# Two slot tiles ahead of the last batch's routing, in an attention, expert and mixing kernel

## The chip, the cores and the metric

The kernel runs on one core of a Trainium2 chip. The metric is the device time of one execution in microseconds (us), as the median of several runs. The engines are named as in the profile: PE (TensorE) multiplies matrices, DVE (VectorE), ACT (ScalarE) and POOL (GpSimd) work on elements, SP (SyncE) only issues transfers. All of them run side by side and wait for one another by semaphores. "PEq", "SPq" and the like are their instruction queues.

## The reference: what is computed

Three stages follow one another on 4 batches of 576 tokens.

```
attention (8 heads of 64):  scores = q k^T / 8;  keep scores >= row maximum - tau;  softmax;  times v
x = heads side by side                                       # 2304 tokens x 512
experts:  logits = x @ w_gate;  e = argmax, or the token before's e while the local gate is >= 0.5 (in one batch)
          out = softmax(logits)[e] * (relu(x @ w1[e]) @ w2[e])          # 8 experts, 512 -> 1024 -> 512
mixing:   theta = x @ w_theta;  zr, zi = x cos, x sin;  y = w_tok_r zr + w_tok_i zi;  u = x + y
          out = u + relu(u @ w_ch)
```

A token goes to exactly one expert. With the reference's inputs the eight experts get 521, 178, 345, 351, 172, 172, 227 and 338 tokens; 354 of expert 0's 521 are in the first three batches. In tiles of 128 rows that is 5, 2, 3, 3, 2, 2, 2 and 3 tiles, 22 in all.

## The kernel before

**Attention** works on 16 pairs of heads (0 to 15, four a batch), each in nine tiles of 128 query rows. In a pair, PE makes the scores, DVE takes row maxima (L417) and masks (L432), ACT the exponentials (L686), DVE the reciprocals of the row sums for three tiles at a time (`recip`, L447), POOL scales those tiles (`norm`, L339), PE turns them (L581) and multiplies by v (L604). Each engine has its order written out by hand in its `pair` function. In the last pairs POOL also splits expert 0's weights, 1024 columns at a time, into a high and a low part (`split_piece`, L65 and L67; the calls are the `pieces` of the last `pair` calls).

**Routing** (`route`) turns the gate's logits into places. Tokens are sorted by expert; each expert gets whole tiles ("slot tiles") of 128 rows. The first three batches are routed during pair 15 (`fresh`, `rows`, `follow`, `count`, `places` with argument 0, then `early`), the last batch after attention (the same with argument 1, then `tile_numbers`, `next_tile`, `next_source`, `all_tiles`, `sources`, `tables`, `weights`). DVE does nearly all of it in one chain; PE has short hops (`rows_pe`, `experts_pe`, `ranks_pe`, and `slots_pe`, 15 or 20 small matmuls that give the token number for each lane of one or more tiles). `hot_lane`, a 128x128 tile for each of 20 groups of tokens, is made by DVE for the first `OWN_LANES` groups and by POOL for the others (`lanes`).

Tile 0 is filled from the first three batches alone, so it can be worked on while the last batch is still being routed. Its rows are fetched from `x_dram` by an indirect DMA of POOL (`fetch`, L1278) with the numbers in `ahead`. Tile 1 is fetched with the second column of `ahead`, after `next_source`; tile 2 with `source`, which `sources` writes for all tiles. The other 23 slots (3 to 25, empty ones too) are gathered by POOL into `stage`, ten places in turn (`gather`), and written by SP to `xs_dram` (L1235), one after another: SP waits for each write to land before it issues the next (L1234). PE's tiles read them back through ACT (L1423).

**Experts** (`experts`): a tile is `transposes_x`, `up` (24 matmuls, L1365), `transposes_h` (L1374), `down` (24 matmuls, L1387). Weights of expert e lie in one of two halves of `w_split`. Expert 0's are split during attention, expert 1's by ACT and DVE (`high`, `low`) beside the first tiles. Experts 2 to 7 are split by POOL in `split` (L1267 high part, L1270 low part): four pieces for `up`, four for `down`, 8 pieces an expert. POOL reaches them only when its 23 gathers are issued. SP loads the raw pieces: expert 2's first four (L1210) before the writes to `xs_dram`, expert 2's last four (L1213) and all others after those writes. From tile 1 on a loop runs: `transposes_h(j)`, `up(j+1)`, `transposes_x(j+2)`, `down(j)`.

**Mixing** is a block of its own; all engines meet ahead of it.

## Time and profile before

| what | us |
|---|---|
| median of 3 runs | 868.75 (868.54 to 869.04) |
| the profiled execution, its own time | 867.34 |
| its span, first to last instruction | 865.6 |
| PE busy | 814.1 (94% of the span) |
| POOL busy | 509.6 (59%) |
| DVE busy | 461.3 (53%) |
| ACT busy | 389.3 (45%) |

In the span attention takes 0 to about 309, the experts 309 to 609, mixing 609 to the end. PE is the busiest engine throughout, so the questions are where it waits, and at which of its two clocks it runs. A busy time says nothing of which wait ends last: for that one reads the bracket at a row's end ("[idle before <-releaser]").

### The profile page before, as it was taken

What the parts mean: (1) busy time and instruction counts of PE and PEld (TensorE: products, weight loads), DVE (VectorE), ACT (ScalarE), POOL (GpSimd) and SP (SyncE); (2) the same over time, 40 slices, a digit from 0 to 9 for tenths busy, and PEclk for the clock granted to TensorE, in tenths of its full rate; (3) what the DMA queues carried; (4) which work ended last, traced back from release to release, by engine and by line L of the source; (5) the groups of instructions that cost most, each with busy time, mean ns of one, the idle gap of its engine ahead of it and who ended that gap; (6) DMA issues with size and microseconds to landing.
All of it is one profiled execution on the core that took longest, in us unless ns stands there. A gap on an engine that the chain in (4) does not pass through costs nothing. (4 is left out here: it accounts for less than half of the span.)

```text
span 865.6 us, 16405 instructions
## 1 busy us (share of the span) xinstructions
PE 814.1 (94%) x5087; PEld 682.8 (79%) x5088; DVE 461.3 (53%) x1078; ACT 389.3 (45%) x669; POOL 509.6 (59%) x464
## 2 busy tenths in 40 slices
PE   6969999999999889999999999998489999999998
PEld 3758878888887657888888888886367899998998
DVE  5748888888888867222122212211286746636622
ACT  2748878787887543221122112121375525434310
POOL 4536776676689837254989999995285605313100
PEclk7879999999999988999999999999699999999999
DMA  6976777768756167765655655650310111100101
GB/s 178 349 177 173 179 190 192 192 170 192 202 129 182 60 220 253 232 208 196 204 196 168 194 179 174 207 193 24 115 49 19 44 56 28 55 28 1 49 9 55
DMA packets 78982, 123.77 MB, mean 143 GB/s; under 512 B 26336, under 2 KB 39904, under 8 KB 78944
## 3 DMA queue, kind: packets, MB, share of 16 engines
q1 hardware_dynamic: 69200, 100.47, 39.9%
q0 software_dynamic: 3552, 11.54, 4.5%
q10 hardware_dynamic: 6192, 11.27, 4.0%
q8 instruction: 21, 0.34, 0.2%
q14 instruction: 17, 0.14, 0.0%
HBM read 70.63 MB, written 24.12 MB: 109 GB/s over the span
## 5 line engine op out<-in xcount | busy, mean ns | idle before, releaser
L339 POOL TENSOR_SCALAR p_ring<-p_ring,xs_nat 128x576 f32<-128x576 f32 x144 | 106.1, 752 | 81.2 <-DVE xs_nat L447 81.2
L417 DVE TENSOR_REDUCE xs_nat<-psum 128x1 f32<-128x576 f32 x144 | 106.0, 750 | 45.6 <-PE psum L546 38.1
L546 PE MATMUL psum<-k_st,q_st 128*128 128x288 f32 x600 | 116.6, 321 | 7.2 <-issue 7.1
L432 DVE SCALAR_TENSOR_TENSOR p_ring<-psum,xs_nat,e_ring 128x576 f32<-128x576 f32 x144 | 114.6, 812 | 16.0 <-PE psum L592 11.4
L1387 PE MATMUL psum<-w_split,h_hi 128*128 (+1 forms) x352 | 118.8, 409 | 3.4 <-DVE h_lo L1484 3.2
L1365 PE MATMUL psum<-w_split,x_hi 128*128 (+1 forms) x352 | 117.0, 403 | 1.3 <-DVE x_lo L1479 0.8
L1270 POOL TENSOR_TENSOR w_split<-w_raw,w_split 128x1024 fp32r<-128x1024 f32 x48 | 115.1, 2397 | 4.0
L686 ACT ACTIVATE e_ring<-psum,xs_nat 128x576 f32<-128x576 f32 x144 | 105.6, 750 | 16.0 <-DVE xs_nat L417 15.1
L704 ACT COPY p_t<-psum 128x512 f32<-128x512 f32 x144 | 84.4, 587 | 37.7 <-PE psum L581 34.6
L546 PEld LDWEIGHTS psum<-k_st,q_st 128*128 128x128 f32 x600 | 86.8, 195 | 18.0 <-DVE p_ring L432 10.4
L1638 POOL TENSOR_TENSOR stage<-g,xs_nat 128x512 f32<-128x512 f32 (+1 forms) x20 | 27.4, 1368 | 110.0 <-ACT xs_nat L1844 110.0
L581 PE MATMUL psum<-ident,p_ring 128*128 128x128 f32 x576 | 89.5, 280 | 1.3 <-POOL p_ring L339 0.6
L1771 PE MATMUL psum<-tok_hi,z_hi 128*128 128x288 f32 x288 | 86.3, 300 | 1.4 <-DVE z_lo L1681 1.4
L1771 PE MATMUL psum<-tok_hi,z_lo 128*128 128x288 f32 x288 | 85.1, 296 | 0.0
L1771 PE MATMUL psum<-tok_lo,z_hi 128*128 128x288 f32 x288 | 85.1, 295 | 0.0
L1387 PEld LDWEIGHTS psum<-w_split,h_hi 128*128 128x128 f32 x352 | 67.9, 193 | 19.4 <-issue 3.7
L1365 PEld LDWEIGHTS psum<-w_split,x_hi 128*128 128x128 f32 x352 | 66.6, 189 | 17.0 <-issue 1.8
L1435 ACT CAST h_hi<-psum 128x1024 fp32r<-128x1024 f32 x22 | 22.4, 1016 | 127.7 <-PE psum L1374 125.3
L581 PEld LDWEIGHTS psum<-ident,p_ring 128*128 128x128 f32 x576 | 69.7, 143 | 9.9 <-issue 7.2
L1387 PE MATMUL psum<-w_split,h_lo 128*128 (+1 forms) x176 | 71.1, 404 | 0.0
L1365 PE MATMUL psum<-w_split,x_lo 128*128 (+1 forms) x176 | 70.0, 398 | 0.0
L604 PE MATMUL psum<-p_t,v_sb 128*64 128x256 f32 (+1 forms) x512 | 69.4, 412 | 0.0
(195 smaller groups left out, 1585.6 us busy)
## 6 DMA issues: line engine op xcount, KB each, us to landing
w_raw<-w_dram SPq DMA_DIRECT2D x48, 512.0 KB
k_st<-k_split SPq DMA_DIRECT2D x60, 320.0 KB, 5.4
q_st<-q_split SPq DMA_DIRECT2D x60, 144.0 KB, 2.5
xs_dram<-stage SPq DMA_DIRECT2D x23, 256.0 KB
ys_dram<-y_nat ACTq DMA_DIRECT2D x22, 256.0 KB
xs_nat<-xs_dram ACTq DMA_DIRECT2D x21, 256.0 KB, 3.3
k_nat<-k_t_dram SPq DMA_DIRECT2D x15, 320.0 KB, 4.2
out_dram<-out_sb SPq DMA_DIRECT2D x32, 144.0 KB, 1.8
```

What stands on the lines that cost most here:

```text
L339: pl.tensor_scalar(t, t, rsum[:, col:col + 1], 1.0, ALU.mult, ALU.mult).then_inc(s_norm, 1)
L417: dve.tensor_reduce(negmax[:, u % 3, 0:1], s_bank[u % 3][:, :, 0:HALF], AX.XY, ALU.max, negate=True).then_inc(s_max, 1)
L432: dve.scalar_tensor_tensor(out=p_tile[u].rearrange("p (a b) -> p a b", a=2), in0=s_bank[u % 3][:, :, 0:HALF], scalar=thresh[:, u % 3:u % 3 ...
L546: mm = pe.matmul(bank[:, x, 0:HALF], lhs, key[:, HALF * x:HALF * x + HALF], start=(j == 0), stop=(j == len(terms) - 1))
L581: mm = pe.transpose(bank[:, t * P:t * P + P], keys[:, t * P:t * P + P], ident[:])
L604: mm = pe.matmul(bank[D * h:D * h + D, 0:COLS[a]], v_sb[m % 2][:, h, t, :], moving, start=(t == 0), stop=(t == KT - 1))
L686: act.activation(e_ring[:, u % 3, :].rearrange("p (a b) -> p a b", a=2), s_bank[u % 3][:, :, 0:HALF], ACT.Exp, bias=negmax[:, u % 3, 0:1], ...
L704: act.copy(dst, src).then_inc(s_free, 1)
L1270: lo = pl.tensor_tensor(w_lo[:, (m + 1) % 2, r // 4, part], raw[:, r % 4, :], w_hi[:, (m + 1) % 2, r // 4, part].bitcast(F32), ALU.subtract)
L1365: mm = pe.matmul(ph[:, half, :], a[:, c, :], rhs.rearrange("p o n -> p (o n)"), start=(n == 0), stop=(n == len(terms) - 1))
L1387: mm = pe.matmul(py, a[:, f, :], rhs.rearrange("p o n -> p (o n)"), start=(n == 0), stop=(n == len(terms) - 1))
L1771: mm = pe.matmul(mix_bank(b, q), a[:, k, c * P:c * P + P], w[:, k, half], start=(t == 0 and i == 0), stop=(t == ST - 1 and i == len(terms) ...
```

## The change

`FIRST_TILES` is 2: tiles 0 and 1 are both filled from the first three batches, both of expert 0 (`first` and `put_first` get a last dimension of 2, `ahead` a third column, expert 0 is padded up to 256 early rows where it has fewer). The token numbers of both come from one hop, and POOL issues both fetches one behind the other. Slot tiles grow from 26 to 27, those fetched directly from 3 to 4, so 23 are still gathered. PE now does both halves of `up(1)` between the hops of the last batch; the hop `next` stands behind the first half of `up(1)`, the hop `sources` behind 12 of the 24 matmuls of `down(0)`. DVE, ACT and the loop (from tile 2 now) follow that order; `tables` comes ahead of `sources` on DVE, and ACT makes the high parts of pieces 2 to 4 of expert 1 ahead of `relu(1)`.

In pair 15 DVE's `fresh` and `rows` of the first three batches stand ahead of the masks of tiles 5 and 6 instead of behind `recip(15, 1)`. POOL's `constants` (three short instructions) stand ahead of a weight piece instead of behind the norms. `OWN_LANES` is 10 instead of 8.

```diff
-SLOTS = (BATCH * SEQ + P - EXPERTS) // P + EXPERTS
+FIRST_TILES = 2
+SLOTS = (BATCH * SEQ + FIRST_TILES * P - EXPERTS) // P + EXPERTS
...
+            if p == PAIRS - 2:
+                routing["pool"]["constants"](pl)
             piece(2)
...
             piece(1)
-            if p == PAIRS - 2:
-                routing["pool"]["constants"](pl)
...
                 row_thresh(i, m, 6)
+                if isinstance(i, int) and 2 * i + m == PAIRS - 1:
+                    routing["vector"]["fresh"](dve, 0)
+                    routing["vector"]["rows"](dve, 0)
                 mask(i, m, 5)
                 mask(i, m, 6)
                 sum_eps(i, m, 1)
                 row_thresh(i, m, 7)
                 recip(i, m, 1)
-                if isinstance(i, int) and 2 * i + m == PAIRS - 1:
-                    routing["vector"]["fresh"](dve, 0)
-                    routing["vector"]["rows"](dve, 0)
...
-    OWN_LANES = 8
+    OWN_LANES = 10
...
-        link(v, v.scalar_tensor_tensor(out=first[:], in0=tile_i[:, 0:EARLY_TT], scalar=0.0, in1=hot[0][:, 0, :],
-                                       op0=ALU.is_equal, op1=ALU.mult))
+        for j in range(FIRST_TILES):
+            link(v, v.scalar_tensor_tensor(out=first[:, :, j], in0=tile_i[:, 0:EARLY_TT], scalar=float(j), in1=hot[0][:, 0, :],
+                                           op0=ALU.is_equal, op1=ALU.mult))
...
-    DIRECT = 3
+    DIRECT = FIRST_TILES + 2
...
-        fetch(x_first, keep["ahead"][:, 0:1], EARLY).then_inc(s_first[0], 16)
+        for j in range(FIRST_TILES):
+            fetch(direct[j], keep["ahead"][:, j:j + 1], EARLY).then_inc(s_first[j], 16)
...
         up(0, halves=range(1), part=range(0, 6))
         hop["experts"](pe, 1)
-        up(0, halves=range(1), part=range(6, 10), ready=False)
+        up(0, halves=range(1), part=range(6, 12), ready=False)
         hop["ranks"](pe, 1)
-        up(0, halves=range(1), part=range(10, 12), ready=False)
         up(0, halves=range(1, 2), ready=False).then_inc(s_up, 1)
+        transposes_x(1, direct[1], s_first[1])
+        transposes_h(0)
+        up(1, halves=range(1))
         hop["next"](pe)
-        transposes_h(0)
+        up(1, halves=range(1, 2), ready=False).then_inc(s_up, 1)
+        down(0, part=range(0, 12))
         hop["sources"](pe)
-        down(0, part=range(0, 4))
-        transposes_x(1, xs[:, 1, :], s_first[1])
-        down(0, part=range(4, 24), ready=False).then_inc(s_done, 1)
+        down(0, part=range(12, 24), ready=False).then_inc(s_done, 1)
+        transposes_x(2, direct[2], s_first[2])
+        transposes_h(1)
         reached(pe, "tables")
-        up(1).then_inc(s_up, 1)
-        transposes_x(2, xs[:, 0, :], s_first[2])
+        up(2).then_inc(s_up, 1)
+        transposes_x(3, direct[3], s_first[3])
+        down(1).then_inc(s_done, 1)
         last = rounds(pe)
-        with pe.Fori(1, last) as j:
+        with pe.Fori(2, last) as j:
```

DVE in pair 15, before (L417 row maximum, L422 threshold, L432 mask, L442 and L447 row sums and reciprocals, L912 to L927 the routing steps):

```order
L422 TENSOR_REDUCE xs_nat<-xs_nat 128x1
L432 SCALAR_TENSOR_TENSOR p_ring,xs_nat<-psum,xs_nat,e_ring 128x576 x2
L442 TENSOR_REDUCE xs_nat<-xs_nat 128x3
L422 TENSOR_REDUCE xs_nat<-xs_nat 128x1
L447 RECIPROCAL xs_nat<-xs_nat 128x3
L913 TENSOR_REDUCE top<-logits 128x15
L914 TENSOR_TENSOR stage<-logits,top 128x120
L916 TENSOR_TENSOR stage<-stage,route_const 128x120
L918 TENSOR_REDUCE fe<-stage 128x15
L924 SCALAR_TENSOR_TENSOR held<-logits,route_const 128x3x5
L927 SCALAR_TENSOR_TENSOR held<-held,fe 128x3x5
L417 TENSOR_REDUCE xs_nat<-psum 128x1
```

The same place in the changed kernel (its lines are one higher):

```order
L423 TENSOR_REDUCE xs_nat<-xs_nat 128x1
L914 TENSOR_REDUCE top<-logits 128x15
L915 TENSOR_TENSOR stage<-logits,top 128x120
L917 TENSOR_TENSOR stage<-stage,route_const 128x120
L919 TENSOR_REDUCE fe<-stage 128x15
L925 SCALAR_TENSOR_TENSOR held<-logits,route_const 128x3x5
L928 SCALAR_TENSOR_TENSOR held<-held,fe 128x3x5
L433 SCALAR_TENSOR_TENSOR p_ring,xs_nat<-psum,xs_nat,e_ring 128x576 x2
L443 TENSOR_REDUCE xs_nat<-xs_nat 128x3
L423 TENSOR_REDUCE xs_nat<-xs_nat 128x1
L448 RECIPROCAL xs_nat<-xs_nat 128x3
L418 TENSOR_REDUCE xs_nat<-psum 128x1
```

Six routing instructions moved ahead of two masks and of the reciprocals for which POOL waits.

PE behind `ranks`, before (L1108 the hops' small matmuls, L1344 the x transposes, L1374 the h transposes, L1365 `up`, L1387 `down`):

```order
L1365 MATMUL psum<-w_split,x_hi 128x512
L1108 MATMUL psum<-put_next,hot_lane 128x2 x20
L1374 MATMUL psum<-ident,h 128x128 x8
L1108 MATMUL psum<-put,hot_lane 128x52 x20
L1387 MATMUL psum<-w_split,h_hi 128x512
...
L1344 MATMUL psum<-ident,xs_nat 128x128 x4
```

The same stretch in the changed kernel (between rows left out stand only more matmuls of the kind above them):

```order
L1355 MATMUL psum<-ident,u 128x128 x4
L1385 MATMUL psum<-ident,h 128x128 x8
L1376 MATMUL psum<-w_split,x_hi 128x512
...
L1116 MATMUL psum<-put_next,hot_lane 128x2 x20
L1376 MATMUL psum<-w_split,x_hi 128x512
...
L1398 MATMUL psum<-w_split,h_hi 128x512
...
L1116 MATMUL psum<-put,hot_lane 128x54 x20
L1398 MATMUL psum<-w_split,h_hi 128x512
...
L1355 MATMUL psum<-ident,xs_nat 128x128 x4
L1385 MATMUL psum<-ident,h 128x128 x8
```

The hop of `put_next` moved behind half of `up(1)`, that of `put` behind all of `up(1)` and half of `down(0)`.

DVE behind the last batch's ranks, before (`put` goes into the hop `sources`, `source` is what comes out of it, `need` is the last of `tables`):

```order
L1033 TENSOR_SCALAR put<-here,route_const 128x20x26
L1484 TENSOR_TENSOR h_lo<-psum,h_hi 128x1024
L994 COPY units<-psum 128x26
L995 SCALAR_TENSOR_TENSOR source<-psum,units 128x26
L1039 TENSOR_TENSOR full<-route_const,ends 1x216
L1041 TENSOR_REDUCE units_row<-full 1x27
L1042 TENSOR_SCALAR slot_expert<-units_row 1x27
L1043 TENSOR_SCALAR rounds<-ends 1x1
L1044 MEMSET need 1x9
L1045 TENSOR_SCALAR need<-ends 1x7
L1479 TENSOR_TENSOR x_lo<-psum,x_hi 128x512
```

The same steps in the changed kernel:

```order
L1041 TENSOR_SCALAR put<-here,route_const 128x20x27
L1047 TENSOR_TENSOR full<-route_const,ends 1x224
L1049 TENSOR_REDUCE units_row<-full 1x28
L1050 TENSOR_SCALAR slot_expert<-units_row 1x28
L1051 TENSOR_SCALAR rounds<-ends 1x1
L1052 MEMSET need 1x9
L1053 TENSOR_SCALAR need<-ends 1x7
L1516 TENSOR_TENSOR w_split<-w_second,w_split 128x1024
L998 COPY units<-psum 128x27
L999 SCALAR_TENSOR_TENSOR source<-psum,units 128x27
L1510 COPY y_nat<-psum 128x512
```

`source`, which frees POOL's fetch and the gathers, moved behind `tables` and one weight piece.

## Rows read from the trace of the kernel before

**Rows 1.** Busy time by stage: window, length, busy us of each engine, clock, DMA.
```profile
343.00:608.80 265.80, 258.95 (x1232) 210.86 (x1232) 58.20 (x66) 51.82 (x62) 201.42 (x118) 0.99 0.55 181
```
**Rows 2.** Timeline of PE: start, length, line, tiles; h transposes of tiles 7 and 18, up(19).
```profile
418.57 1.03 PE L1374 MATMUL psum<-ident,h 128*128 128x128 f32 x8
...
556.03 1.03 PE L1374 MATMUL psum<-ident,h 128*128 128x128 f32 x8
557.27 0.49 PE L1365 MATMUL psum<-w_split,x_hi 128*128 x1 [0.20 <-issue]
```
**Rows 3.** Timeline of POOL: first split of expert 2's down weights, last of expert 7's up.
```profile
408.13 1.05 POOL L1267 TENSOR_SCALAR w_split<-w_raw 128x1024 fp32r<-128x1024 f32 x1 [11.17 <-DMA w_raw<-w_dram]
...
554.52 2.40 POOL L1270 TENSOR_TENSOR w_split<-w_raw,w_split 128x1024 fp32r<-128x1024 f32 x1
```
**Rows 4.** Group of POOL by line, 408 to 573 us: busy, mean ns, idle before.
```profile
L1267 POOL TENSOR_SCALAR w_split<-w_raw 128x1024 fp32r<-128x1024 f32 x44 | 46.2, 1049 | 20.2 <-DMA w_raw<-w_dram 11.2 <-issue 5.3 <-POOL w_split L1270 2.3
```
**Rows 5.** Timeline of SP's queue, from six starts up to 405 us: writes still to come.
```profile
337.06 65.66 SPq L1235 DMA_DIRECT2D xs_dram<-stage  x23
...
343.54 59.18 SPq L1235 DMA_DIRECT2D xs_dram<-stage  x22
...
351.01 51.71 SPq L1235 DMA_DIRECT2D xs_dram<-stage  x20
...
384.48 18.23 SPq L1235 DMA_DIRECT2D xs_dram<-stage  x9
...
402.39 0.33 SPq L1235 DMA_DIRECT2D xs_dram<-stage  x1
404.66 0.39 SPq L1213 DMA_DIRECT2D w_raw<-w_dram  x1
```
**Rows 6.** Timeline of SP's queue, 270 to 430 us: expert 2's first raw pieces.
```profile
329.53 1.76 SPq L1210 DMA_DIRECT2D w_raw<-w_dram  x4
```
**Rows 7.** Timelines of DVE and POOL: last step of `sources`, first gather.
```profile
327.48 0.18 DVE L995 SCALAR_TENSOR_TENSOR source<-psum,units 128x26 int32<-128x26 f32 x1
...
329.65 0.95 POOL L1278 DMA_INDIRECT stage<-x_dram,source  x1 [0.76 <-DVE need L1045]
```
**Rows 8.** Source view of L1278: issue to landing of the fetches.
```profile
DMA to landing us min/median/max: 3.7/4.2/5.3
```
**Rows 9.** Timeline of PE, 309 to 345 us: tile 0, hops, tile 1.
```profile
310.62 0.66 PE L1344 MATMUL psum<-ident,u 128*128 128x128 f32 x4 [1.45 <-DMA u<-x_dram,ahead]
...
312.90 0.77 PE L1365 MATMUL psum<-w_split,x_hi 128*128 128x512 f32 x1 [0.82 <-DVE x_lo L1479]
...
321.78 1.23 PE L1108 MATMUL psum<-put_next,hot_lane 128*128 128x2 bf16 x20 [0.84 <-DVE put_next L1023]
...
325.39 1.83 PE L1108 MATMUL psum<-put,hot_lane 128*128 128x52 bf16 x20 [0.47 <-DVE put L1033]
...
343.02 1.09 PE L1374 MATMUL psum<-ident,h 128*128 128x128 f32 x8 [0.68 <-ACT h L1431]
344.37 0.49 PE L1365 MATMUL psum<-w_split,x_hi 128*128 x1 [0.26 <-issue]
```
**Rows 10.** Busy time by window as in rows 1, by the clock.
```profile
312.90:316.20 3.30, 3.30 (x11) 2.26 (x11) 1.54 (x3) 1.38 (x2) 0.00 (x0) 0.52 1.00 377
...
322.80:333.20 10.40, 9.75 (x49) 7.61 (x47) 7.14 (x21) 4.97 (x7) 5.37 (x5) 0.51 0.43 132
```
**Rows 11.** Timelines of DVE, POOL and PE in pair 15.
```profile
289.71 0.78 DVE L914 TENSOR_TENSOR stage<-logits,top 128x120 f32<-128x120 f32 x1
...
298.89 0.28 DVE L958 TENSOR_TENSOR sel<-psum,hot 128x120 f32<-128x120 f32 x1 [0.46 <-PE psum L1096]
...
305.72 0.16 DVE L995 SCALAR_TENSOR_TENSOR ahead<-psum,units 128x1 int32<-128x1 f32 x1
...
300.29 4.90 POOL L1133 TENSOR_SCALAR hot_lane<-bf_lane,place 128x128 bf16<-128x128 bf16 x7 [0.42 <-DVE place L962]
...
293.03 0.74 PE L1073 MATMUL psum<-ident,held 128*3 128x128 f32 x5 [2.25 <-DVE held L927]
```

More of the change, by code:

```diff
@@ L976, in early @@
         v.wait_ge(s_hop, 4)
-        token(v, keep["ahead"][:, 0:1], first_at, 1, "first")
+        token(v, keep["ahead"][:, 0:FIRST_TILES], first_at, FIRST_TILES, "first")
     def behind(v):
         link(v, v.tensor_copy(before[:], tiles_of[0][:, :, EARLY_TT - 1]))
-        link(v, v.tensor_scalar(missing[0:1, :], counts_at[0][0:1, 0:1], -1.0, float(P), ALU.mult, ALU.add))
-        link(v, v.scalar_tensor_tensor(out=before[0:1, 0:1], in0=missing[0:1, :], scalar=0.0,
-                                       in1=tiles_of[0][0:1, 0, EARLY_TT - 1:EARLY_TT], op0=ALU.max, op1=ALU.add))
+        for j, at in enumerate((slice(0, 1), slice(32, 33))):
+            link(v, v.tensor_scalar(missing[at, :], counts_at[0][at, 0:1], -1.0, float(P * j + P), ALU.mult, ALU.add))
+            link(v, v.tensor_scalar(missing[at, :], missing[at, :], 0.0, float(P), ALU.max, ALU.min))
+            link(v, v.tensor_tensor(before[at, 0:1], missing[at, :], tiles_of[0][at, 0, EARLY_TT - 1:EARLY_TT], ALU.add))
         link(v, v.memset(others_last[:], 1.0))
@@ L1020, in next_tile @@
     def next_tile(v):
-        link(v, v.scalar_tensor_tensor(out=put_next[:, :, 0], in0=tile[:], scalar=1.0, in1=C["token"],
+        n = float(FIRST_TILES)
+        link(v, v.scalar_tensor_tensor(out=put_next[:, :, 0], in0=tile[:], scalar=n, in1=C["token"],
                                        op0=ALU.is_equal, op1=ALU.mult))
-        link(v, v.tensor_scalar(put_next[:, :, 1], tile[:], 1.0, C["number"], ALU.is_equal, ALU.mult), "put_next")
+        link(v, v.tensor_scalar(put_next[:, :, 1], tile[:], n, C["number"], ALU.is_equal, ALU.mult), "put_next")
     def next_source(v):
         v.wait_ge(s_hop, 8)
-        token(v, keep["ahead"][:, 1:2], next_at, 1, "next")
+        token(v, keep["ahead"][:, FIRST_TILES:FIRST_TILES + 1], next_at, 1, "next")
     def all_tiles(v):
@@ L1305, in pool @@
         reached(pl, "next")
-        fetch(xs[:, 1, :], keep["ahead"][:, 1:2]).then_inc(s_first[1], 16)
+        at = FIRST_TILES
+        fetch(direct[at], keep["ahead"][:, at:at + 1]).then_inc(s_first[at], 16)
         reached(pl, "source")
-        fetch(xs[:, 0, :], keep["source"][:, 2:3]).then_inc(s_first[2], 16)
+        fetch(direct[at + 1], keep["source"][:, at + 1:at + 2]).then_inc(s_first[at + 1], 16)
         reached(pl, "tables")
@@ L1347, in parity @@
         def parity(j):
-            if isinstance(j, int) and j == 0:
+            if isinstance(j, int) and j < FIRST_TILES:
                 return 0, 1
@@ L1393, in tensor @@
         pe.sem_inc(s_up, 1)
[L1394 removed]
+        transposes_x(0, direct[0], s_first[0])
         hop["rows"](pe, 1)
@@ L1449, in scalar @@
         high(0)
-        high(1)
         relu(0)
-        high(2)
+        x_high(1)
         h_high(0)
-        high(3)
-        x_high(1)
-        for r in range(4, PIECES):
+        for r in range(1, 5):
             high(r)
         relu(1)
+        for r in range(5, PIECES):
+            high(r)
         x_high(2)
-        load(3)
+        h_high(1)
         store(0)
+        relu(2)
+        x_high(3)
+        load(4)
+        store(1)
         reached(act, "tables")
         last = rounds(act)
-        with act.Fori(1, last) as j:
+        with act.Fori(2, last) as j:
             h_high(j)
@@ L1514, in vector @@
         r["places"](v, 1)
+        r["tile_counts"](v)
+        x_low(1)
         r["tile_numbers"](v)
         r["next_tile"](v)
+        h_low(0)
         r["next_source"](v)
         r["all_tiles"](v)
-        h_low(0)
+        r["tables"](v)
+        low(0)
         r["sources"](v)
-        r["tables"](v)
-        x_low(1)
+        y_out(0)
+        x_low(2)
+        for n in range(1, 4):
+            low(n)
+        h_low(1)
         r["weights"](v)
-        y_out(0)
-        for n in range(5):
-            low(n)
-        x_low(2)
+        low(4)
+        x_low(3)
         for n in range(5, PIECES):
             low(n)
+        y_out(1)
         last = rounds(v)
-        with v.Fori(1, last) as j:
+        with v.Fori(2, last) as j:
             h_low(j)
@@ L1961, in build @@
         xs = sb("xs_nat", [P, 2, DIM], F32)
-        s_first = [sem(f"e_first{m}") for m in range(3)]
+        s_first = [sem(f"e_first{m}") for m in range(FIRST_TILES + 2)]
         s_xst = [sem(f"s_xst{m}") for m in range(2)]
@@ L2029, in build @@
                     groups = attention_programs[-1]
-                    experts_programs = experts(nc, d, place, sem, psum, ident, keep, w, feed, early, late, xs, zeros, s_first,
+                    experts_programs = experts(nc, d, place, sem, psum, ident, keep, w, feed, early, late, xs, x_first, s_first,
                                                s_xst, s_free, groups, routing)
```

26 lines of the change are left out of this document (15 added, 11 removed).

## The prediction

> **What bounds the kernel now.** I read the busy time by stage first: in the expert stage, 343 to 608.8 us, PE is busy for 259.0 of 265.8 us at a granted clock of 0.99, POOL for 201.4 [rows 1]. A stage so full on one engine looks as if every microsecond that PE gains at its start came out at its end. So the second view is PE's timeline at the places where a new expert's weights are first used. A tile costs PE 12.50 us: tile 7 turns its h at 418.57, tile 18 at 556.03, eleven tiles later [rows 2]. From one h transpose to the next `up` it is normally 0.8 us; behind 556.03 it is 1.24, with 0.20 us idle, and `up(19)` starts at 557.27 [rows 2]. Tile 19 is the first of expert 7 (5+2+3+3+2+2+2 = 19 tiles lie ahead of it), and POOL's last split of that expert's up weights ends at 554.52 + 2.40 = 556.92 [rows 3]. PE waits there for POOL, if only just. Followed backwards, POOL has no slack: from 408.13 to 572.4 it splits 44 pieces (x44), 1.05 us for the high and 2.40 for the low part, and of its idle time only 11.2 us is a wait on another's work, the DMA at the very start [rows 3, 4]. That start, the first down piece of expert 2 at 408.13, waits for a raw piece that SP issues at 404.66, behind the last of 23 writes to `xs_dram` [rows 3, 5]. The writes are a serial queue from 337.06 to 404.66 [rows 5], begun when the first gather lands; the gather is issued at 329.65, once DVE has written `source` (327.48 + 0.18 = 327.66) and the tables [rows 7].
>
> Two chains therefore meet at 557: PE's own work, and hop `sources`, gathers, 23 writes, raw pieces, 12 half experts on POOL. What the change is worth is the smaller of the two gains.
>
> **PE's chain.** Pair 15 first. Before, PE waits 2.25 us until 293.03 for `held` [rows 11]. The six moved instructions took 3.45 us (289.43 to 292.88), with 0.78 for L914 beside POOL's norms; an instruction of the same 120 elements took 0.28 later [rows 11]. In the new place they start at about 287.7, when POOL has one norm left and then waits for the very reciprocals that now come later. At 0.28 for the long ones they cost 1.8 us: masks 5 and 6 move back by 1.8, PE now idles for mask 5 ahead of scores 8 instead of for `held`, and `rows_pe` starts at about 291.7, 1.3 us earlier. At the old durations it would be 293.4, 0.4 later, so this part lies between -1.3 and +0.4; POOL's own norms and weight piece have room for 1.8 us, since it waited for both groups of reciprocals anyway. I take -1.3, because POOL's wait is what the steps would lie beside. Then POOL's lanes: 7 took 4.90 [rows 11], now 5 take 3.5 and DVE makes two more (0.35 each), the longer side ending about 0.4 us earlier relative to the chain. Two more instructions of 0.17 for `first` go against that and are in it. Together `ahead`, at 305.72 before [rows 11], comes 1.7 earlier, tile 0's rows 1.7 earlier, and `behind`, four short DVE instructions longer (0.7 us), is hidden behind the last x_tmp copy but for a few tenths. `up(0)` starts at 311.0 instead of 312.90 [rows 9].
>
> The Trainium skill, page "SBUF — State Buffer", section "Who interferes with whom", says that a DVE instruction with two SBUF inputs and a GpSimd one that reads SBUF shut each other out for a whole instruction. By it alone the steps would cost their short times (the -1.3 above); by the old row they would not (+0.4).
>
> From there: `up(0)` 5.6 us (24 of a tile's 48 matmuls), 1.4 more since six of them fall in a stretch at half clock as before (granted 0.52 from 312.9 to 316.2 [rows 10]), the hops `experts` and `ranks` 0.9: 318.9. Then relu, x copy and x_lo: 1.1 for relu, then 1.35 as between 343.02 and 344.37 [rows 9]: `up(1)` at 321.4. Then up 5.6, hop `next` 1.23, down 5.6, hop `sources` 1.83 [rows 9], tx, th and the x_lo wait 1.7 (the x transposes now stand directly ahead of th), up 5.6, tx 0.36, down 5.6, in all 27.5: the loop reaches th(2) at 348.9. Before that is 418.57 less five tiles, 356.1 [rows 2]. So PE arrives 7.2 us early: 1.9 from pair 15 and 5.3 from waits and half-speed matmuls of the old prologue (0.84, 0.47 and 0.68 us idle [rows 9], 10.4 us at a clock of 0.51 from 322.8 to 333.2 [rows 10], of which I charge nothing to the new one, since the same relu and x_lo waits at 341.7 to 344.4 did not lower the clock).
>
> The number of tiles doesn't grow: expert 0 has 354 early tokens, more than 256, so no padding. The extra slot adds a zero write in attention and 20 to 40 elements to some DVE instructions, hidden or under 0.1 us.
>
> **POOL's chain.** The hop `sources` moved behind `up(1)` and half of `down(0)`: 321.4 + 5.6 + 1.23 + 2.8 + 1.83 = 332.9, `source` at 333.3 instead of 327.66, 5.6 later. Behind it on POOL stand one fetch and then the gathers; 1.5 us after `source` the first gather is issued, 334.8 instead of 329.65. `tables` comes earlier relative to `source`, so SP's four raw pieces (2 MB, issued at 329.53 before [rows 6]) go at about 329 again, now with no gather beside them.
>
> Before, the first gather took 7.4 us to land (329.65 to 337.06), beside those 2 MB; the fetches take 3.7 to 5.3, median 4.2 [rows 8]. So the first write starts at 339.0 (338.5 to 342.2), 2.0 us late. The first two writes took 6.48 and 5.40 us, the first one behind the raw pieces in SP's own queue and both beside a backlog of gathers; the first three together 13.95 [rows 5]. From the fourth (351.01) to the fifteenth (384.48), with about one gather each, a write takes 3.04, and the last one, alone, 2.27 [rows 5]. In the changed kernel the raw pieces are out of the way when the first write starts, and the gathers are issued one in 1.25 us without a backlog. Three writes then cost between 9.1 (3.04 each) and 13.95; nearest is 3.04 with more gathers than usual beside it, and I take 3.5 each, 10.5: the fourth starts at 349.5 instead of 351.01, 1.5 us early. The other 20 have the same work beside them and keep their 53.65 us. So the raw pieces, POOL's 408.13, and everything to 556.92 come 1.5 us early. Bounds: first write at 338.5 and 3.04 each gives -3.4; landing after 7.4 us and old lengths gives +5.1.
>
> **The sum.** PE reaches `down(7)` at 418.2 and waits for POOL to about 420.7; it keeps 4.7 us of its 7.2 until tile 19 and loses them to 1.5 there. Mixing starts 1.5 us earlier and is unchanged. Profiled execution: 867.34 - 1.5 = 865.8. The median of the runs is 868.75, 1.4 above it; the same difference gives **867.2 us**.
>
> **Rivals.**
> 1. PE's gain arrives whole: 868.75 - 7.2 = 861.5. The share of PE in rows 1 speaks for it; the 0.20 us idle right behind POOL's 556.92 speaks against. It would take a write queue 7 us shorter, beyond my bound. 6%.
> 2. Slower: the write queue starts late and keeps its lengths, because the gathers, whose issue isn't thinned, collide with it all the same. First write 2.0 us late, everything behind it too: 870.8. It decides at the first three writes: above 11.95 us in all, the kernel is slower. The DMA share of 1.00 at 377 GB/s from 312.9 to 316.2 [rows 10] shows how weights fill it; that POOL's gathers no longer meet 2 MB of them speaks against. 13%.
> 3. PE's half clock returns in the longer prologue. In rows 10 it lasted 10.4 us at 0.51 after 0.84 us idle and small matmuls; the same stretch ahead of hop `sources` puts it 5 us later, the first gather too, and the fourth write at 354.5: +3.5, 872.2. The dense `up` on both sides of hop `next` speaks against. 7%. The Trainium skill, "TensorE: Matmul & The Clock Gate", section "What's actually happening", has the half rate as the default that activity lifts; no run here yet shows how the new row of hops counts.
> 4. Pair 15 gives nothing: `source` comes 1.8 later and so do the writes, 0.3 late: 869.1. 16%.
>
> **Chances.** The forecast has 58%, its own range 865.3 to 868.5. About 0.2%, 1.7 us, is what a measurement of this kernel tells from no change. The forecast at -1.5 lies just inside that; half of its weight and rival 1 beyond it, and some of the forecast's upper end goes with rival 4 to "same". Faster 0.42, same 0.38, slower 0.20. Range 864.3 to 870.8.
>
> **What would show it.** Right: `up(19)` follows POOL's last up piece of expert 7 within 0.5 us, behind an idle of 3 us or more, and PE also waits at `down(7)`; th(2) near 349; first write near 339, the first raw piece of expert 2's down weights near 403. Pair 15: L914's successor at 0.3 to 0.5 us, `ahead` near 304. Wrong: no idle at `up(19)` (then PE's chain is the bound, rival 1), or raw pieces at 406 or later (rival 2 or 3; the clock of 321 to 333 tells them apart).

## The result, and the profile after

| | before | changed |
|---|---|---|
| median of 18 runs each, on the same chip | 869.78 us (866.13 to 872.23) | 872.75 us (868.74 to 877.65) |
| the profiled execution, its own time | 867.34 | 869.99 |
| its span | 865.6 | 868.1 |

The ratio is 1.0039 with a 95% interval of [1.0022, 1.0056]: the changed kernel is 0.4% slower, 3.0 us by the medians. The forecast was 867.2 us, 1.5 us faster than before; 872.75 lies outside the range up to 870.8. A ratio here and below is an estimate from all runs of both kernels, not the quotient of the two medians, from which it can differ by up to 0.2%.

Where in the span does the time go? Busy time by stage of the changed kernel: window, length, busy us of PE, PEld, DVE, ACT and POOL, clock, DMA share, GB/s.

```profile
307.30:352.80 45.50, 41.26 (x210) 31.50 (x211) 26.14 (x70) 15.83 (x19) 17.79 (x20) 0.89 0.71 240
352.80:612.90 260.10, 248.25 (x1172) 201.43 (x1170) 55.01 (x63) 48.86 (x58) 198.95 (x116) 0.99 0.54 179
612.90:868.10 255.20, 237.06 (x1568) 218.66 (x1568) 138.79 (x237) 104.00 (x174) 79.45 (x61) 0.97 0.13 42
```

The first window starts where PE has ended attention and waits for tile 0's rows, the second where it reaches the h transposes of tile 2, the third where the expert stage ends, each at the same point of the program in both kernels. The same windows in the kernel before are 46.90, 252.80 and 256.70 us long; its second is:

```profile
356.10:608.90 252.80, 246.12 (x1173) 200.53 (x1171) 52.19 (x60) 48.87 (x58) 196.57 (x114) 0.99 0.54 178
```

So the prologue starts 1.9 us earlier and is 1.4 shorter, PE's loop is 7.3 us longer with the same matmuls (1172 against 1173), and mixing is 1.5 shorter with the same 1568 matmuls.

PE's timeline of the changed kernel: `up(0)`, h transposes of tile 0, `up(1)`, h transposes of tile 2 and 7, and the two places where it waits for POOL.

```profile
311.59 0.79 PE L1376 MATMUL psum<-w_split,x_hi 128*128 128x512 f32 x1
...
323.20 1.09 PE L1385 MATMUL psum<-ident,h 128*128 128x128 f32 x8 [0.68 <-ACT h L1446]
324.57 0.47 PE L1376 MATMUL psum<-w_split,x_hi 128*128 128x512 f32 x1 [0.27 <-DVE x_lo L1498]
...
352.56 1.04 PE L1385 MATMUL psum<-ident,h 128*128 128x128 f32 x8
...
416.15 1.03 PE L1385 MATMUL psum<-ident,h 128*128 128x128 f32 x8
426.37 0.79 PE L1398 MATMUL psum<-w_split,h_hi 128*128 x1 [3.16 <-POOLq L1284]
...
561.16 0.50 PE L1376 MATMUL psum<-w_split,x_hi 128*128 x1 [1.62 <-POOLq L1284]
```

PE reaches tile 2's h at 352.56, 3.5 us earlier than before (356.1, which is 418.57 of [rows 2] less five tiles). It reaches tile 7's h at 416.15 against 418.57 [rows 2], still 2.4 early: tile 2 took 13.6 us instead of 12.5, which no other profile of this order shows. Then it waits 3.16 us at `down(7)`, the first use of expert 2's down weights, and 1.62 at `up(19)`, the first of expert 7's. That `up` starts at 561.16 against 557.27, 3.9 us late. Behind the first wait PE also runs at half clock, which the windows after it show:

```profile
426.40:429.40 3.00, 3.00 (x7) 2.42 (x8) 0.00 (x0) 0.00 (x0) 1.76 (x2) 0.50 0.50 180
429.40:445.00 15.60, 15.60 (x74) 12.68 (x74) 2.61 (x3) 2.52 (x3) 14.81 (x9) 1.00 0.52 167
```

Seven matmuls in 3.0 us there, against 74 in 15.6 us afterwards. So tile 7, from its h transposes to those of tile 8, takes 17.3 us instead of 12.5: 3.2 of the 4.8 are the wait, nearly all of the rest is the half clock behind it.

POOL's timeline of the changed kernel: the fetch of tile 2, the first gather, expert 2's first down piece, expert 7's last up piece.

```profile
336.45 0.95 POOL L1287 DMA_INDIRECT xs_nat<-x_dram,source  x1 [5.54 <-DVE source L999]
337.70 0.95 POOL L1287 DMA_INDIRECT stage<-x_dram,source  x1 [0.30 <-issue]
...
412.15 1.05 POOL L1276 TENSOR_SCALAR w_split<-w_raw 128x1024 fp32r<-128x1024 f32 x1 [10.93 <-DMA w_raw<-w_dram]
...
558.46 2.35 POOL L1279 TENSOR_TENSOR w_split<-w_raw,w_split 128x1024 fp32r<-128x1024 f32 x1
```

And SP's queue: expert 2's first raw pieces, the writes still to come from four starts, its last raw pieces.

```profile
332.70 1.76 SPq L1219 DMA_DIRECT2D w_raw<-w_dram  x4
342.63 63.92 SPq L1244 DMA_DIRECT2D xs_dram<-stage  x23
...
347.03 59.53 SPq L1244 DMA_DIRECT2D xs_dram<-stage  x22
...
351.10 55.46 SPq L1244 DMA_DIRECT2D xs_dram<-stage  x21
...
355.84 50.71 SPq L1244 DMA_DIRECT2D xs_dram<-stage  x20
...
408.51 1.92 SPq L1222 DMA_DIRECT2D w_raw<-w_dram  x4
```

Read it against [rows 3, 5, 7]. The first gather is 8.0 us later (337.70 against 329.65), the first write 5.6 (342.63 against 337.06), expert 2's raw pieces 3.9 (408.51 against 404.66), POOL's first split of them 4.0 (412.15 against 408.13), expert 7's last up piece ends at 560.81 instead of 556.92, 3.9 late. POOL's own 44 pieces are as long as before:

```profile
L1276 POOL TENSOR_SCALAR w_split<-w_raw 128x1024 fp32r<-128x1024 f32 x44 | 46.2, 1050 | 20.0 <-DMA w_raw<-w_dram 10.9 <-issue 6.8 <-POOL w_split L1279 2.3
```

4.0 us at the end of the expert stage less the 1.5 of mixing are the 2.5 us of the span (868.1 against 865.6). The change doesn't touch mixing, and the time from PE's last wait for `h_lo`, just before the end of the expert stage, to the end of the span is 264.2 to 269.1 us in the fourteen profiles of this document. The 1.5 lies within that spread, so I don't count it as an effect of the change.

In this profile pair 15 did what was forecast. DVE's timeline of the changed kernel there, and `ahead`:

```profile
286.71 0.27 DVE L914 TENSOR_REDUCE top<-logits 128x15 f32<-128x120 f32 x1
287.01 0.29 DVE L915 TENSOR_TENSOR stage<-logits,top 128x120 f32<-128x120 f32 x1
...
303.82 0.16 DVE L999 SCALAR_TENSOR_TENSOR ahead<-psum,units 128x2 int32<-128x2 f32 x1
```

L915 is the 0.78 us of [rows 11]'s L914; now it takes 0.29, and `ahead` comes 1.9 us earlier. That is one execution against one. Over all profiles of this document `ahead` stands at 302.5 to 306.0 in the nine kernels with pair 15's edits and at 304.7 to 306.9 in the five without: 1.4 us earlier in the mean, with a spread that is larger.

### The profile page after: what moved, and what is told of

Its sections match the earlier page's. It is cut to its first block and busy times, and to the rows that moved or that the text cites. A ratio compares the mean times of both kernels' runs of the same rounds, so it can differ in the third digit from the quotient of the medians.

```text
span 868.1 us, 16350 instructions
## 1 busy us (share of the span) xinstructions
PE 813.3 (94%) x5087; PEld 680.2 (78%) x5088; DVE 461.6 (53%) x1085; ACT 389.2 (45%) x669; POOL 507.4 (58%) x463
## 5 line engine op out<-in xcount | busy, mean ns | idle before, releaser
L1376 PE MATMUL psum<-w_split,x_hi 128*128 (+1 forms) x352 | 119.6, 409 | 2.9 <-POOLq L1284 1.6
L687 ACT ACTIVATE e_ring<-psum,xs_nat 128x576 f32<-128x576 f32 x144 | 105.6, 749 | 13.4 <-DVE xs_nat L418 12.7
```

Source lines behind the costliest of these rows:

```text
L687: act.activation(e_ring[:, u % 3, :].rearrange("p (a b) -> p a b", a=2), s_bank[u % 3][:, :, 0:HALF], ACT.Exp, bias=negmax[:, u % 3, 0:1], ...
L1376: mm = pe.matmul(ph[:, half, :], a[:, c, :], rhs.rearrange("p o n -> p (o n)"), start=(n == 0), stop=(n == len(terms) - 1))
```

## The experiments

Each was compared with the kernel before on its own chip (26 to 32 runs of that), so ratios from one chip can be set side by side: 1 to 4 share one chip, 5 to 8 another, 9 to 12 a third. Theory W, made after the result: PE's chain is 3 to 4 us shorter, but the hop `sources` moved behind more PE work, so gathers, writes, expert 2's down pieces and POOL come later, and PE pays at `down(7)` and `up(19)`. The rivals: pair 15's edits cost the time (B); the half clock of the prologue does (C); PE's longer prologue itself or mixing costs it, and the writes are beside the point (P); leaving out gathers and writes gains by less DMA traffic, whatever the tiles (E).

**1. The changed kernel once more** (no edit).

> The changed kernel once more, for a second profile of it and as the partner of the others on this chip. Theory W (the queue of 23 writes to xs_dram, started by the hop sources, feeds POOL's splits, and these set the time at which up(19) starts): about 3.0 us slower than before, and the start of POOL's first down piece of expert 2 (412.15 in the first profile, 408.13 before) moves with the end of the hop sources and with the half-clock stretch ahead of it; if that stretch is shorter in this profile by x us, the first gather is x/2 earlier. Theory P (PE's longer prologue itself, or the mixing stage's clock, costs the time): same time, but no relation between 412.15 and the end.

Measured: 872.0 us, ratio 1.0045 [1.0019, 1.0071]. Its profiled execution was the shortest of its 12 (866.52), and shows how far one execution can be from another. First comes the window of `up(0)` in the first profile of the changed kernel (columns as in the stage windows above):

```profile
311.00:325.00 14.00, 13.05 (x52) 9.27 (x50) 5.32 (x20) 3.55 (x5) 3.51 (x5) 0.67 0.79 298
```

The same window of this execution:

```profile
311.00:325.00 14.00, 13.05 (x79) 9.89 (x78) 6.86 (x21) 6.93 (x8) 3.50 (x5) 0.93 0.75 282
```

And timelines of this execution: POOL's first gather, SP's writes from the first and from the fourth, POOL's first down piece, PE at `down(7)`:

```profile
333.99 0.95 POOL L1287 DMA_INDIRECT stage<-x_dram,source  x1 [0.30 <-issue]
...
338.84 65.12 SPq L1244 DMA_DIRECT2D xs_dram<-stage  x23
...
352.36 51.61 SPq L1244 DMA_DIRECT2D xs_dram<-stage  x20
...
409.50 1.04 POOL L1276 TENSOR_SCALAR w_split<-w_raw 128x1024 fp32r<-128x1024 f32 x1 [11.57 <-DMA w_raw<-w_dram]
...
423.66 0.79 PE L1398 MATMUL psum<-w_split,h_hi 128*128 x1 [5.22 <-POOLq L1284]
```

At 0.93 instead of 0.67 PE does 79 matmuls instead of 52 in the same 14 us, and the first gather is issued at 333.99 instead of 337.70. So the half clock is real: of these 3.7 us it accounts for 2.8 (from the first matmul of `up(0)` to the next x transposes, 10.3 us in the first profile and 7.5 here); the other 0.9 was there already at `up(0)`. But even here POOL's first down piece is late (409.50 against 408.13 before), PE waits 5.2 us for it, and PE's wait for `h_lo` at the end of the stage ends 1.1 us later than before (599.27 against 598.21). With a good clock in the prologue the expert stage was still not shorter. The whole execution says less: its 866.52 us is about the 866.72 that the kernel before has as its median on this chip; mixing was 1.9 us shorter in it than in the profile before. The Trainium skill, "TensorE: Matmul & The Clock Gate", section "What's actually happening", says that the number of matmuls at the low clock, as a kernel starts, varies from run to run of one kernel; these two profiles show the like in mid-kernel, with 0.67 and 0.93.

**2. Pair 15's edits alone**, on the kernel before: `fresh` and `rows` ahead of masks 5 and 6, `constants` ahead of the piece, `OWN_LANES` 10. Nothing else of the change.

```diff
+            if p == PAIRS - 2:
+                routing["pool"]["constants"](pl)
             piece(2)
...
+                if isinstance(i, int) and 2 * i + m == PAIRS - 1:
+                    routing["vector"]["fresh"](dve, 0)
+                    routing["vector"]["rows"](dve, 0)
                 mask(i, m, 5)
...
+    OWN_LANES = 10
```

> The kernel before with only the edits of pair 15 (fresh and rows ahead of masks 5 and 6, the constants ahead of a weight piece, ten lanes on DVE). Theory W: the changed kernel's trace showed tile 0's rows 1.7 us earlier; here hop sources, the first gather (329.65 before), the writes and POOL's 408.13 all come 1.7 to 2 us earlier and so does the end: 1.9 us faster than before. Theory P: PE gains the same 1.9 us at the start and, if PE's own chain is the bound, also at the end; so this run tells whether the edits of pair 15 or the second tile cost the time, not W from P. If pair 15's edits are what costs, it is slower by 3 us.

Measured: 868.22 us, ratio 1.0000 [0.9974, 1.0026]. B falls: these edits alone don't slow the kernel by 0.4%. The 1.9 us that were expected of them aren't seen either; they would be 0.22%, which the interval just doesn't exclude. SP's queue of this kernel:

```profile
327.99 1.76 SPq L1210 DMA_DIRECT2D w_raw<-w_dram  x4
335.00 69.48 SPq L1235 DMA_DIRECT2D xs_dram<-stage  x23
406.48 1.92 SPq L1213 DMA_DIRECT2D w_raw<-w_dram  x4
```

And PE's waits for POOL (us in total, times, longest), the first at `up(19)`, the second at `down(7)`:

```profile
PE psum L1365 <- POOLq L1275: 3.0, 1, 3.0
PE psum L1387 <- POOLq L1275: 1.1, 1, 1.1
```

The first gather (328.10) was 1.55 us and the first write 2.1 us earlier than in [rows 5, 7], but the 23 writes took 69.48 instead of 65.66, so that the raw pieces came 1.8 later and PE waited. What lengthened them in this execution is not settled; one profile can't tell an effect of the edit from the spread between executions.

**3. The tiles alone**: the changed kernel with pair 15, `constants` and `OWN_LANES` as before (a part of the diff; the lines added here are taken out at the other place).

```diff
                 recip(i, m, 1)
+                if isinstance(i, int) and 2 * i + m == PAIRS - 1:
+                    routing["vector"]["fresh"](dve, 0)
+                    routing["vector"]["rows"](dve, 0)
...
+    OWN_LANES = 8
```

> The changed kernel with pair 15 as before (the two tiles alone). Theory W: everything behind pair 15 is 1.9 us later than in the changed kernel, the first gather near 339.6 instead of 337.70, the end 1.9 us later than the changed kernel, 4.9 us slower than before. If pair 15's edits are what costs: equal to before or faster.

Measured: 871.33 us, ratio 1.0037 [1.0009, 1.0064], beside 1.0045 for the whole change on this chip. So the slowdown is of the tiles' part; the further 1.9 us that were expected without pair 15's edits didn't show. POOL's first down piece starts at 414.52, PE waits 4.9 us at `down(7)` and 0.6 at `up(19)`.

**4. Fewer writes in the queue**: the changed kernel without the gathers and writes of the slots that are empty with these inputs (22 to 26). It leaves out that part of the computation, which other inputs would need: 18 writes instead of 23.

```diff
+USED = 22
...
-        for j in range(DIRECT, SLOTS):
+        for j in range(DIRECT, USED):
             sp.wait_ge(s_got[(j - DIRECT) % NG], 16 * ((j - DIRECT) // NG) + 16)
...
-        for j in range(DIRECT, SLOTS):
+        for j in range(DIRECT, USED):
             gather(j)
```

> The changed kernel with the 5 slots (22 to 26) that hold no tokens with these inputs neither gathered nor written: 18 gathers and 18 writes instead of 23. Theory W: the write queue ends 5 x 2.1 = 10.4 us earlier, POOL's first down piece of expert 2 starts near 402 instead of 412.15, PE's waits for POOL at down(7) (3.2 us) and up(19) (1.6 us) go, and the kernel is 4.8 us faster than the changed one, 1.8 us faster than before. Theory P: the writes are beside the point, the time stays 3 us above before.

Measured: 861.61 us, ratio 0.9922 [0.9890, 0.9953]. SP's queue in this kernel:

```profile
344.22 50.07 SPq L1245 DMA_DIRECT2D xs_dram<-stage  x18
396.55 1.93 SPq L1223 DMA_DIRECT2D w_raw<-w_dram  x4
```

The first write started even later than in the changed kernel (344.22), yet the raw pieces come at 396.55. POOL's first down piece starts at 400.17, and the view of PE's waits from 345 to 590 us is empty: no wait for POOL is left. This speaks for W and against B, C and P: the end of the write queue comes 12 us forward, PE's order is untouched, its prologue is as slow as in the changed kernel (10.1 us from the first matmul of `up(0)` to the next x transposes), and +0.4% turns into -0.8%. Rival E is left, since five gathers and five writes are gone; 5 and 7 deal with it.

**5. The same on the kernel before** (slots 22 to 25 left out, 19 writes, with the same part of the computation missing). The diff is that of 4.

> The kernel before with the slots 22 to 25, empty with these inputs, neither gathered nor written (19 writes instead of 23). Theory W (the serial writes feed POOL's splits; where POOL is late PE waits, and a long wait is followed by a stretch at half clock): in the profile of before PE waited 0.2 us for POOL, in other runs perhaps more, so this gains 0.2 to 2 us on before, far from the 6.7 us (0.78%) that the two tiles without their 5 empty slots gained; the difference of the two kernels is what the second early tile is worth once the writes are out of the way, 4 to 7 us. Rival E (leaving out gathers and writes is worth 6 us by itself, by less DMA traffic, whatever the tiles): 5 us faster than before or more.

Measured: 865.17 us, ratio 0.9966 [0.9945, 0.9986]. E would have given this kernel 5 us or more; it gained 0.3%, less than half of what 4 gained. The 0.3% suggest that POOL's chain held the kernel before as well. Its profile shows little of that, 0.20 us of idle at `up(19)` [rows 2]; whether other executions of it wait longer wasn't measured. With the queue short in both, the change is worth 0.9922 / 0.9966 = 0.9956 (two chips, so without an interval).

**6. The hop `sources` earlier**: in the changed kernel, ahead of all of `down(0)` on PE, and `sources` ahead of `tables` on DVE.

```diff
-        down(0, part=range(0, 12))
         hop["sources"](pe)
-        down(0, part=range(12, 24), ready=False).then_inc(s_done, 1)
+        down(0).then_inc(s_done, 1)
...
-        r["tables"](v)
-        low(0)
         r["sources"](v)
+        r["tables"](v)
+        low(0)
```

> The changed kernel with the hop sources ahead of down(0) instead of in its middle, and DVE's sources ahead of tables. Theory W: hop, source and first gather come 2.8 us earlier than in the changed kernel at the same clock (334 to 335 after a long half-clock stretch, near 331 after a short one), POOL's first down piece of expert 2 as much, and the end 2.8 to 4 us earlier than the changed kernel: 0 to 1 us from before. Rival E or P: same as the changed kernel, 3 to 4 us slower than before.

Measured: 873.17 us, ratio 1.0065 [1.0038, 1.0093]: no cure, where 2.8 to 4 us less than the changed kernel were expected. POOL and SP of this kernel:

```profile
334.30 0.97 POOL L1287 DMA_INDIRECT xs_nat<-x_dram,source  x1 [2.81 <-DVE source L999]
336.03 1.81 POOL L1287 DMA_INDIRECT stage<-x_dram,source  x1 [0.76 <-DVE need L1053]
...
335.91 1.84 SPq L1219 DMA_DIRECT2D w_raw<-w_dram  x4
345.02 64.50 SPq L1244 DMA_DIRECT2D xs_dram<-stage  x23
```

The first gather is issued 1.7 us earlier (336.03), but in the same microsecond as 2 MB of raw pieces, and lands 9.0 us later instead of 4.9. So an earlier `source` is worth nothing if `tables`, which releases the raw pieces, comes right behind it. The kernel before had a milder form (7.4 us, [rows 5, 7]).

**7. Expert 2's down pieces between the writes**: the changed kernel, with each of the four raw pieces issued by SP behind write 16, 18, 20 and 22 instead of all behind the last.

```diff
             sp.dma_start(xs_d[j], staged[:, (j - DIRECT) % NG, :]).then_inc(s_put, 16)
+            if j - DIRECT in (15, 17, 19, 21):
+                piece(2, 4 + (j - DIRECT - 15) // 2)
...
-        for r in range(4, PIECES):
-            piece(2, r)
```

> The changed kernel with all 23 gathers and writes, but SP issues expert 2's last four raw pieces behind the 16th, 18th, 20th and 22nd write instead of behind the 23rd (this holds for routings in which expert 0 has fewer than some 15 tiles). Theory W: POOL goes on from expert 2's up pieces to its down pieces nearly without a wait, some 9 us earlier than 409 to 412, the waits at down(7) and up(19) go and the kernel is 9 to 10 us faster than the changed one, 6 us (0.7%) faster than before, as without the empty slots. Rival E: the traffic is the same, so the time stays at the changed kernel's, 3 to 4 us above before.

Measured: 861.43 us, ratio 0.9931 [0.9906, 0.9957]. Nothing is left out. SP's queue and POOL of this kernel:

```profile
339.30 51.68 SPq L1244 DMA_DIRECT2D xs_dram<-stage  x16
391.03 0.43 SPq L1222 DMA_DIRECT2D w_raw<-w_dram  x1
393.00 2.84 SPq L1244 DMA_DIRECT2D xs_dram<-stage  x2
395.89 0.43 SPq L1222 DMA_DIRECT2D w_raw<-w_dram  x1
...
401.04 1.05 POOL L1276 TENSOR_SCALAR w_split<-w_raw 128x1024 fp32r<-128x1024 f32 x1 [0.45 <-POOL w_split L1279]
```

PE's waits from 345 to 590 us (us in total, times, longest), the whole view:

```profile
PE psum L1376 <- POOLq L1284: 0.5, 1, 0.5
```

POOL goes from the up pieces to the down pieces at 401.04 with 0.45 us idle, in place of 10.93 of waiting for `w_raw`. The waits at `down(7)` and `up(19)` are gone; the one left, at `up(7)`, is 0.5 us. The traffic is the same as in the changed kernel, so E can't be the reason. This is the strongest evidence for W: only the place of four loads in SP's queue differs.

**8. The same edit, with the diff of 7, on the kernel before.**

> The same edit of SP in the kernel before. Theory W: only 0.2 to 2 us faster than before, since there PE's own chain and POOL's meet within 1 us at up(19). Rival E: no change.

Measured: 864.68 us, ratio 0.9960 [0.9941, 0.9979], on the same chip as 7. It has no wait for POOL, so PE's chain is the bound in both, and the change is worth about 3 us: 861.43 - 864.68 = -3.25 by the medians, -2.5 by the ratios. That fits the 3.5 us by which PE reached tile 2 earlier.

**9. The first four raw pieces out of the gathers' way**: in the changed kernel, expert 2's up pieces behind write 6, 8, 10 and 12 instead of ahead of the writes.

```diff
-        for r in range(4):
-            piece(2, r)
...
+            if j - DIRECT in (5, 7, 9, 11):
+                piece(2, (j - DIRECT - 5) // 2)
```

> The changed kernel, but SP issues expert 2's first four raw pieces behind the 6th, 8th, 10th and 12th write instead of ahead of the first gathers. Theory W: the first gather lands 4 to 4.5 us after its issue instead of 4.9 (9.0 where both were issued together), the first three writes take 9 to 11 us instead of 13.2; but each piece between two writes costs its 2 us there, as it did between the late writes of e7, so the queue ends within 2 us of the changed kernel's, and the time is within 2 us of it (3 to 4 us slower than before). If only the first landing mattered, it is 3 us faster than the changed kernel.

Measured: 875.69 us, ratio 1.0093 [1.0062, 1.0124]. SP's queue of this kernel:

```profile
343.04 21.23 SPq L1242 DMA_DIRECT2D xs_dram<-stage  x6
364.31 0.42 SPq L1219 DMA_DIRECT2D w_raw<-w_dram  x1
366.14 3.77 SPq L1242 DMA_DIRECT2D xs_dram<-stage  x2
...
381.84 0.48 SPq L1219 DMA_DIRECT2D w_raw<-w_dram  x1
386.81 25.26 SPq L1242 DMA_DIRECT2D xs_dram<-stage  x11
415.51 1.92 SPq L1222 DMA_DIRECT2D w_raw<-w_dram  x4
```

This run was expected within 2 us of the changed kernel, and missed: 1.0093 is 0.5% above the 1.0039 of that kernel. Nor are the first three writes at the 9 to 11 us expected. But it measures the disputed cost by itself. No raw piece is near, but the first gather (issued at 337.87) still lands after 5.2 us, and the first three writes still take 13.2 us (starts at 343.04 and 356.28), as in the changed kernel. So the 2 MB aren't needed to make them slow. What is left beside them is POOL's own gathers, one every 1.25 us against a write every 4: in the changed kernel the last of that run of gathers is issued at 352.73, and the fourth write, from 355.84, takes 3.2 us. No run spaced the gathers out, so this cause is argued and not shown. And the pieces now cost the queue 1.8 to 5 us each, so the down pieces come 7.0 later than in the changed kernel (415.51) and PE waits 9.4 us at `down(7)`, and 1.2 at `up(7)`.

**10 and 11. Each part of the change alone, with the queue out of the way**: 10 is the kernel before with the diffs of 2 and 7, 11 the changed kernel with the diffs of 3 and 7.

> The kernel before with the edits of pair 15, and the down pieces between the writes as in e7 and e8. With POOL's chain out of the way PE's is the bound, and pair 15 alone brings its 1.7 to 1.9 us: 0.4% + 0.2% = 0.6% faster than before. If the edits of pair 15 are worth nothing even to PE (a longer half-clock stretch behind them), 0.4% as e8.

> The changed kernel with pair 15 as before, and the down pieces between the writes. With PE's chain as the bound the second early tile brings 3 to 5 us on e8 less 1.9 against e7: 0.5% faster than before. Rival: the tiles bring nothing and e7's gain over e8 is pair 15's, then 0.4% as e8.

Measured: 865.20 us, ratio 0.9972 [0.9950, 0.9994], and 862.24 us, ratio 0.9939 [0.9917, 0.9962]. Neither has a wait for POOL between 345 and 600 us. The tiles are the gain: on this one chip 11 lies 3 us below 10, although 10 has pair 15's edits and 11 has not. 10 was expected 0.6% faster than before and is 0.3% faster. For pair 15 one must set chips side by side: 0.9972 beside the 0.9960 of 8 on the old order, and 0.9931 (7) beside 0.9939 on the new one, +0.1% and -0.1%. A gain of 1.4 us, as `ahead` has it in the mean, would be 0.16%: the intervals neither show nor exclude it.

**12. Both cures**: the diffs of 4 (empty slots left out, as there) and 7 together, with the raw pieces behind write 12, 14, 16 and 18.

```diff
+            if j - DIRECT in (11, 13, 15, 17):
+                piece(2, 4 + (j - DIRECT - 11) // 2)
```

> The changed kernel without the 5 empty slots and with the down pieces behind the 12th, 14th, 16th and 18th write: both cures of the write queue at once. PE's chain was the bound in e4 and e7 already, except 0.55 us of waiting at up(7) in e7: 0 to 1 us faster than e7, 0.7 to 0.8% faster than before. If POOL's chain still held either of them back, 3 us faster than both.

Measured: 861.10 us, ratio 0.9918 [0.9889, 0.9946], no wait for POOL. Beside 4 (0.9922) and 7 (0.9931) it brings nothing that can be measured: with either cure PE's chain is the bound, and the second has nothing to take away. Of the kernels that compute everything, 7 and 11 are the fastest and not to be told apart; both beat the kernel before and the changed one. The order of 7 is written for these inputs: an expert 0 of some fifteen tiles or more would need rows that SP writes behind a raw piece which itself waits for expert 0 to end. That limit is argued, not tried.

## Why the prediction was wrong

Right: two chains meet, the change is worth the smaller of the two gains, and POOL's is the smaller (4, 5, 7 and 8 show it). The waits stand at `down(7)` and `up(19)` as forecast, and `up(19)` starts 0.35 us after POOL's piece ends. Their sizes were off: 3.2 us at `down(7)` for 2.5, and 1.6 at `up(19)` where 3 or more was forecast. About 1.7 us of half clock behind the first wait and 1.1 us in tile 2, which I didn't have, stood in place of the rest. Pair 15's durations were right (0.29 for 0.78); that `ahead` came 1.9 earlier for a forecast 1.7 is in part luck, with the spread between executions given above. Right was also the way from `up(1)` to the first gather (13.1 us for 13.4). A slip without effect: the chain to `up(19)` has ten half experts on POOL, not 12.

The step that failed is the sum of POOL's chain, forecast at -1.5 and measured at +4.0 at its first down piece. Term by term:

| term | forecast | changed kernel | off |
|---|---|---|---|
| `up(1)` starts | 321.4 | 324.57 | +3.2 |
| from there to the first gather | 13.4 | 13.1 | -0.3 |
| gather to first write | 4.2 | 4.9 | +0.7 |
| first three writes | 10.5 | 13.2 | +2.7 |
| fourth write to raw pieces, to POOL | 57.1 | 56.3 | -0.8 |
| together | | | +5.5 |

- **The half clock of the prologue**, +3.2. I gave `up(0)` 1.4 us for six slow matmuls, and charged nothing for the 10.4 us at 0.51 of [rows 10], since they stood in a part of the prologue that was rewritten. In the changed kernel `up(0)` and both hops take 10.3 us, from 311.59 to the x transposes at 321.93, where I had 7.9: that is 2.4 of the 3.2. Another 0.6 is a later start of `up(0)` (311.59 for 311.0; the five `held` transposes ahead of it took 1.20 us, for 0.74 before), and 0.2 lies behind it. The windows of it, slow and then full:

```profile
310.00:320.20 10.20, 9.74 (x32) 6.70 (x33) 4.99 (x19) 1.62 (x3) 0.77 (x2) 0.50 1.01 371
320.30:324.00 3.70, 3.02 (x19) 2.42 (x18) 0.27 (x1) 1.50 (x2) 2.64 (x4) 1.00 0.48 179
```

Ahead of it stand small transposes and waits of 1.69 and 0.84 us, much as before ([rows 9] has 1.45 and 0.82 there). Rival 3 named this with 7%, and its 872.2 us is near the 872.75, but it put the half clock at 321 to 333, where the changed kernel's profile has the full one; the number agrees by luck. In this profile it was the largest term of the miss. It isn't there in every execution: from the first matmul of `up(0)` to the x transposes it takes 7.5 to 10.3 us in the nine profiles of this order, and three of them (1, 7 and 11) are at my 7.9 or within 0.4 of it.
- **The first three writes**, +2.7 (and +0.7 for the landing). I took [rows 5]'s 13.95 us as the price of 2 MB beside the gathers, and went near 3.04 each because the 2 MB would be gone. They were gone (issued at 332.70, 9.9 us ahead of the first write), and the writes took 13.2. Experiment 9 shows that they take that with no raw piece near at all, and in the nine profiles of this order they take 12.2 to 14.3 us, never near 10.5. This term alone was enough to turn the sign: in experiment 1's execution `up(1)` is 0.5 us ahead of the forecast, the three writes take 13.5 (338.84 to 352.36), and POOL's first down piece is at 409.50, 1.4 later than before, where I had 1.5 earlier. Rival 2 said that the writes stay slow because the gathers collide with them all the same, with 13%; that they stay slow is shown, that the gathers do it is not. Its deciding point, 11.95 us, was right: 13.2 lies above. Its 870.8 us, 2.0 above before, lacks the half clock; the medians are 3.0 apart.

PE's own chain was mis-sized as well: 7.2 us early at tile 2 forecast, 3.5 measured, 3.2 of the difference being the same late `up(1)`. That didn't decide, since POOL's chain was the bound. With POOL's chain out of the way (experiments 7 and 8) the change brings about 3 us, not 7.2.

Rival 4 (pair 15 gives nothing, 869.1 us) isn't settled. No median shows a gain of it (2, 3, 10, 11), but `ahead` comes earlier in the mean, by an amount that is too small for these intervals.

## What to carry to other kernels

When work of the busiest engine moves ahead of a short step of a serial chain, follow that chain to its end before you count the gain: here one short hop, 8.9 us later (334.31 against 325.39), held back gathers, 23 serial writes and eleven half experts of weights. Don't explain a slow queue by the one large neighbour that you can remove, unless a stretch without it shows the fast price; bound it by the slow price. And when a change with a clear local gain comes out slower, look for the other chain: moving four weight loads in a queue turned +0.4% into -0.7%.

## What was unexpected of the hardware

- A write of 256 KB to DRAM, awaited before the next, took 2.27 us as the last of its queue [rows 5], 3.04 with about one gather beside it, and 4.4 in the mean of the first three, beside gathers issued every 1.25 us. The Trainium skill, "DMA: Bandwidth & Descriptors", section "Anatomy of one DMA — SWDGE (gpsimd) path", puts about 2.0 us of a DMA issued by GpSimd down to a fixed part, mostly the write's receipt, and gives 436 GB/s for the rest. These writes are SP's; taken over to them that makes 2.6 us, an estimate, near the 2.27 and far from the 4.4.
- From the issue of the first gather to its landing, which starts the first write, it took 4.8 to 5.3 us in the eight kernels of the new order in which SP's loads weren't issued with it, 6.9 to 7.5 in the five of the old order, where they were, and 9.0 when 2 MB of weight loads were issued in the same microsecond (experiment 6).
- Two executions of one kernel granted PE 0.67 and 0.93 over the same 14 us, and the first gather moved by 3.7 us; a single profile of a kernel with such a prologue is worth that much less.
- A wait of 3.16 us for POOL was followed by 3 us at a clock of 0.50; the 1.62 us at `up(19)` wasn't followed by such a stretch. The wait of 2.96 us in experiment 2, at `up(19)`, was: the clock was 0.54 over the next 6.7 us.
